# Two routings and a tail on one core: earlier and half strided gate matmuls, fewer warming transposes, and a bank of its own for the last logits group

## The reference

```python
# 1: linear attention, batch 4, 8 heads, 768 steps, head size 48
for t in range(S):
    cur = einsum('bhd,bhe->bhde', u * k[t], v[t])
    y[t] = einsum('bhd,bhde->bhe', r[t], state + cur)
    state = w * state + einsum('bhd,bhe->bhde', k[t], v[t])
# x: 3072 rows of 384
# 2: mixture of experts, E = 8, hidden 1024, for rows with x @ w_skip > 0 only
e = argmax(x @ w_gate); gate = softmax(x @ w_gate)[e]
x = x + gate * (relu(x @ w1[e]) @ w2[e])
# 3: a second such layer for every row, without the addition of x
out = gate * (relu(x @ w1b[e]) @ w2b[e])
```

## Time and profile before

| | us |
|---|---|
| median of 3 runs | 567.01 (564.94 to 568.14) |
| the profiled execution | 566.76 |
| its span, first to last instruction | 564.9 |
| TensorE busy | 535.0 |
| VectorE busy | 377.9 |
| ScalarE busy | 267.1 |
| GpSimd busy | 257.0 |

### The profile page before, as it was taken

The page is one execution under the profiler, slowest core; times in us unless marked ns, Lnnn a source line. Parts: engine busy times, 40 slices in busy tenths (PEclk is TensorE's granted clock), DMA queues, the critical chain, the costliest instruction groups (busy, mean ns, idle before and its releaser), DMA issues. The chain is left out here.

```text
span 564.9 us, 15988 instructions
## 1 busy us (share of the span) xinstructions
PE 535.0 (95%) x5511; PEld 506.8 (90%) x5512; DVE 377.9 (67%) x825; ACT 267.1 (47%) x718; POOL 257.0 (45%) x374
## 2 busy tenths in 40 slices
PE   4899999996899999999998899999999999999994
PEld 4789988994899999999986899999999999999993
DVE  4788888885698878888855646564756464647331
ACT  0333333333667656778743546362635452626230
POOL 5887787765145554444412342423332413324241
PEclk9999999996799999999998899999999999999998
DMA  9788889857278876784478524544454544111101
GB/s 154 130 179 161 162 161 173 164 192 275 84 247 266 259 231 188 240 263 131 117 233 297 189 71 149 167 149 143 164 173 150 166 142 159 38 48 42 41 2 41
DMA packets 114129, 89.59 MB, mean 159 GB/s; under 512 B 80672, under 2 KB 104931, under 8 KB 114080
## 3 DMA queue, kind: packets, MB, share of 16 engines
q1 hardware_dynamic: 105744, 73.96, 46.5%
q0 software_dynamic: 7776, 14.82, 9.5%
q10 hardware_dynamic: 560, 0.20, 0.2%
HBM read 80.44 MB, written 13.27 MB: 166 GB/s over the span
## 5 line engine op out<-in xcount | busy, mean ns | idle before, releaser
L777 DVE TENSOR_TENSOR w_lo<-w_raw,w_hi 128x384 fp32r<-128x384 f32 (+1 forms) x224 | 130.1, 608 | 4.8 <-ACT w_hi L772 3.6
L772 ACT CAST w_hi<-w_raw 128x384 fp32r<-128x384 f32 (+1 forms) x224 | 120.2, 566 | 4.2 <-issue 4.2
L1134 PE MATMUL e_ps_h<-e_x_hi,w_hi 128*128 128x192 f32 (+3 forms) x384 | 119.3, 311 | 1.0 <-DVE e_x_lo L1342 0.5
L1136 PE MATMUL e_ps_h<-e_x_hi,w_lo 128*128 128x192 f32 (+3 forms) x384 | 119.3, 311 | 0.0
L1135 PE MATMUL e_ps_h<-e_x_lo,w_hi 128*128 128x192 f32 (+3 forms) x384 | 119.3, 311 | 0.0
L1384 DVE SCALAR_TENSOR_TENSOR e_h_lo<-e_ps_h,e_h_hi 128x128 fp32r<-128x128 f32 (+1 forms) x192 | 70.4, 397 | 42.6 <-ACT e_h_hi L1290 36.0
L1134 PE MATMUL e_ps_y<-w_hi,e_h_hi 128*128 128x384 f32 x272 | 95.6, 352 | 0.0
L1136 PE MATMUL e_ps_y<-w_hi,e_h_lo 128*128 128x384 f32 x272 | 91.4, 336 | 0.0
L1135 PE MATMUL e_ps_y<-w_lo,e_h_hi 128*128 128x384 f32 x272 | 91.4, 336 | 0.0
L1134 PEld LDWEIGHTS e_ps_h<-e_x_hi,w_hi 128*128 128x128 f32 x384 | 72.7, 189 | 2.7 <-DVE e_x_lo L1342 1.4
L1135 PEld LDWEIGHTS e_ps_h<-e_x_lo,w_hi 128*128 128x128 f32 x384 | 72.7, 189 | 1.0
(11 more groups left out here) (208 smaller groups left out, 936.2 us busy)
## 6 DMA issues: line engine op xcount, KB each, us to landing
w_raw<-in_moe_w_dram SPq DMA_DIRECT2D x32, 1536.0 KB, 6.4
r_in<-in_r_dram SPq DMA_DIRECT2D x24, 192.0 KB, 3.2
k_in<-in_k_dram SPq DMA_DIRECT2D x24, 192.0 KB, 3.9
v_in<-in_v_dram SPq DMA_DIRECT2D x24, 192.0 KB, 3.9
x_rows<-rows SPq DMA_DIRECT2D x24, 192.0 KB, 3.4
w_raw<-x_rows SPq DMA_DIRECT2D x4, 768.0 KB, 8.7
e_late_x<-x_rows SPq DMA_DIRECT2D x2, 768.0 KB, 6.7
x_in<-x_rows,e_ent_in POOLq DMA_INDIRECT x33, 3.0
```

Source lines behind the costliest of these rows:

```text
L772: act.copy(self._of(self.hi1[par], self.hi2[par], n), self._of(self.raw1[par], self.raw2[par], n)).then_inc(self.hi_done[par], 1)
L777: eng.tensor_tensor(self._of(self.lo1[par], self.lo2[par], n), self._of(self.raw1[par], self.raw2[par], n), self._of(self.hi1[par], self.h ...
L1134: pe.matmul(o, s_hi, m_hi, start=(k == 0), stop=False)
L1136: return pe.matmul(o, s_lo, m_hi, start=False, stop=(k == last))
```

## The change

GpSimd's four fills move ahead of the constants. `stay_warm` has 2 turns in layer one and 3 in layer two in place of 6. VectorE makes the first half of `words_by_column` ahead of `starts`. ScalarE copies only this half into `gate_words`, which is half as large. TensorE's gate matmuls move ahead of its wait for `routed`; they begin with the second half of the tiles, read from `words_by_column` at a stride of 24 elements, and go on with the first half from `gate_words`. `start_spans` moves behind the turn of the second tile. In the tail the last group has halves of the bank `ps_y[1]` and a second `lT` tile; its `logitsT` stands directly behind that of the group before.

```diff
-        gate_words = sb("gate_words", [P, TILES, 3, NCOL], BF16)
+        gate_words = sb("gate_words", [P, TILES // 2, 3, NCOL], BF16)
...
+            if m == 0:
+                for row in fresh_rows:
+                    pool.memset(row[:], 0.0).then_inc(made, 1)
             exact = dict(allow_small_or_imprecise_dtypes=True)
...
             if m == 0:
-                for row in fresh_rows:
-                    pool.memset(row[:], 0.0).then_inc(made, 1)
...
-            stay_warm(pe, ident, ps_spare[:], 6)
+            stay_warm(pe, ident, ps_spare[:], 3 if m else 2)
...
-            for n, half in enumerate(HALVES):
-                act.wait_ge(gates_spread, n + 1)
-                act.copy(gate_words[:, half, :, :].rearrange("p i w c -> p i (w c)"), words_by_column[:, :, :, half].rearrange("p w c i -> p i (w c)")).then_inc(gates_aside, 1)
+            act.wait_ge(gates_spread, 1)
+            act.copy(gate_words[:].rearrange("p i w c -> p i (w c)"), words_by_column[:, :, :, HALVES[0]].rearrange("p w c i -> p i (w c)")).then_inc(gates_aside, 1)
...
+            def spread_gates(half):
+
+                wide = [P, 3, NCOL, half.stop - half.start]
+                dve.tensor_tensor(words_by_column[:, :, :, half], col_is[:, :, half].unsqueeze(1).to_broadcast(wide), pieces[:, :, half].unsqueeze(2).to_broadcast(wide), ALU.mult).then_inc(gates_spread, 1)
...
+            dve.wait_ge(gates_split, 5)
+            spread_gates(HALVES[0])
             if m == 0:
                 link(dve.tensor_tensor(over_short[:], seen[:, :, TILES - 1:TILES].to_broadcast([P, E, MOST]), short_limit[:].unsqueeze(1).to_broadcast([P, E, MOST]), ALU.is_gt))
...
-            dve.wait_ge(gates_split, 5)
-            for half in HALVES:
-                wide = [P, 3, NCOL, half.stop - half.start]
-                dve.tensor_tensor(words_by_column[:, :, :, half], col_is[:, :, half].unsqueeze(1).to_broadcast(wide), pieces[:, :, half].unsqueeze(2).to_broadcast(wide), ALU.mult).then_inc(gates_spread, 1)
+            spread_gates(HALVES[1])
             dve.wait_ge(starts_made, 5 if m == 0 else 4)
...
-            lT = sb("lT", [P, P])
+            lT = [sb(f"lT{n}", [P, P]) for n in range(2)]
...
+            ps_lT = lambda g: ps_y[1][:, 0:P] if g == XG else ps_x[0][:, 0:P]
+            ps_l = lambda g: ps_y[1][:, P:2 * P] if g == XG else ps_x[1][:, 0:P]
...
+            pe.wait_ge(gates_spread, 2)
+            for i in range(TILES // 2, TILES):
+                pe.matmul(ps_gates, row_hot[:, :, i], words_by_column[:, :, :, i], start=(i == TILES // 2), stop=False)
+            pe.wait_ge(gates_aside, 1)
+            for i in range(TILES // 2):
+                ins = pe.matmul(ps_gates, row_hot[:, :, i], gate_words[:, i, :, :], start=False, stop=(i == TILES // 2 - 1))
+            ins.then_inc(gates_placed, 1)
             pe.wait_ge(routed, 1)
-            start_spans(pe)
 
             for n in range(4):
                 pe.transpose(ps_h[n][:, P * WHOLE:P * WHOLE + P], ident[:], ident[:])
-            for n, some in enumerate(HALVES):
-                pe.wait_ge(gates_aside, n + 1)
-                for i in range(some.start, some.stop):
-                    ins = pe.matmul(ps_gates, row_hot[:, :, i], gate_words[:, i, :, :], start=(i == 0), stop=(i == TILES - 1))
-            ins.then_inc(gates_placed, 1)
             turn_x(0, 0)
...
                 turn_x(0, n)
+                if n == 1:
+                    start_spans(pe)
...
-                    if g:
+                    if 0 < g < XG:
                         pe.wait_ge(lT_out, g)
-                    else:
+                    elif g == 0:
                         pe.wait_ge(x_lo_done, X * units_run + X)
...
                 for g in range(XG + 1):
-                    logitsT(g)
+                    if g < XG:
+                        logitsT(g)
                     if g + 2 < XG + 1:
                         turn(g + 2)
+                    if g == XG - 1:
+                        logitsT(XG)
                     logits_of(g)
...
                 for g in range(XG + 1):
-                    logitsT_out(g)
+                    if g < XG:
+                        logitsT_out(g)
                     if g + 2 < XG + 1:
                         turned_copy(act, g + 2, 0)
+                    if g == XG - 1:
+                        logitsT_out(XG)
                     logits_out(g)
```

More of the change, by code:

```diff
@@ L717, in _ @@
             dve.tensor_copy(table[:, 0:NCOL, 0], ids[:]).then_inc(routed, 1)
-        return row_hot, gate_words, gates_aside, routed
+        return row_hot, words_by_column, gates_spread, gate_words, gates_aside, routed
 class Weights:
@@ L783, in wait_split, with moe @@
         eng.wait_ge(self.lo_done[k][par], (self.N1, self.N - self.N1)[k] * (pair + 1))
-def moe(nc, both, block, m, W, rows, out_rows, ident, USED, table, starts, x_in, y_rows, w_g, lg, ent_last, row_hot, gate_words, gates_aside, routed):
+def moe(nc, both, block, m, W, rows, out_rows, ident, USED, table, starts, x_in, y_rows, w_g, lg, ent_last, row_hot, words_by_column, gates_spread, gate_words, gates_aside, routed):
     tag = f"e{m}"
@@ L865, in moe @@
         pairs = E // 2
-        TILES, NCOL = gate_words.shape[1], gate_words.shape[3]
-        HALVES = [slice(0, TILES // 2), slice(TILES // 2, TILES)]
+        NCOL, TILES = words_by_column.shape[2:]
         gates_placed = sem("gates_placed")
@@ L1226, in logitsT @@
                         for b in range(SIZES[g]):
-                            ins = pe.matmul(ps_x[0][GW * b:GW * b + GW, 0:P], w_g[:, c, :], xT[g % 2][b][:, P * c:P * c + P], start=(c == 0), stop=(c == DC - 1), skip_group_check=True)
+                            ins = pe.matmul(ps_lT(g)[GW * b:GW * b + GW, :], w_g[:, c, :], xT[g % 2][b][:, P * c:P * c + P], start=(c == 0), stop=(c == DC - 1), skip_group_check=True)
                     ins.then_inc(lT_ready, 1)
@@ L1232, in logits_of @@
                     pe.wait_ge(lT_out, g + 1)
-                    if g:
+                    if 0 < g < XG:
                         pe.wait_ge(l_out, g)
-                    pe.transpose(ps_x[1][:, 0:P], lT[:], ident[:]).then_inc(l_ready, 1)
+                    pe.transpose(ps_l(g), lT[g == XG][:], ident[:]).then_inc(l_ready, 1)
                 turn(0)
@@ L1315, in logitsT_out @@
                     act.wait_ge(lT_ready, g + 1)
-                    act.copy(lT[:], ps_x[0][:, 0:P]).then_inc(lT_out, 1)
+                    act.copy(lT[g == XG][:], ps_lT(g)).then_inc(lT_out, 1)
                 def logits_out(g):
@@ L1322, in logits_out @@
                     dst = y_logits[:] if i is None else lg[:, BY * i:BY * i + BY, COL:COL + E]
-                    act.copy(dst, ps_x[1][:, 0:P].rearrange("p (b w) -> p b w", w=w_g.shape[2])[:, 0:SIZES[g], COL:COL + E]).then_inc(l_out, 1)
+                    act.copy(dst, ps_l(g).rearrange("p (b w) -> p b w", w=w_g.shape[2])[:, 0:SIZES[g], COL:COL + E]).then_inc(l_out, 1)
                 turned_copy(act, 0, 0)
```

## The result

The changed kernel takes 563.86 us (median of 5 runs, 562.42 to 564.08) against 567.01 of the kernel before, run beside it: a ratio (of the runs as a whole, not of the two medians) of 0.9947 with an interval of 0.9922 to 0.9972. Two later sets of runs of the same kernel gave 0.9914 [0.9874, 0.9955] and 0.9932 [0.9912, 0.9952]. So it is faster, by 3.2 us between the medians, about half of the 6.1 us that the sum promised. Its profiled execution took 563.98 us, 0.1 above its median, with a span of 562.3 where the kernel before has 564.9.

A forecast was written before the change was run, and what follows sets the result against it. TensorE, busy 95% of the span, bounds the kernel; gains lie in both routings and the tail. Terms -3.2 - 2.4 + 0.3 + 0.1 - 0.2 - 0.9 = -6.3, less 0.2 given back: -6.1, median 560.9 us; range 559.4 to 564.3.

The forecast's parts named there:

- the clock rival: The clock falls early or rises late in one layer, slowing routing and expert start: 562.5 to 564.3 us; chance 0.20.
- Part 1, layer one: Routing of layer one: fewer warming transposes bring the reduce from 149.75 to 146.5, bound by VectorE's list; -3.2 us.
- Part 1, layer two: Routing of layer two: fewer warming transposes bring the reduce from 321.81 to 319.4; -2.4 us.
- 11 at the lower and 13 at the higher clock: Layer two's 24 warming transposes: the clock rises among them, so they take 3.9 us and end at 315.05.
- the case that the text priced at 1.1: Layer two: the clock does not rise in the 24 transposes, L626 ends at 320.6, and the gain is 1.1 us.
- Part 2: Gate words half copied, half read strided at 0.21 and 0.245 us a matmul: hidden in layer one, +0.3 us in two.
- The slower rival: TensorE at 1.2 GHz reads strided tiles at half the rate: 575 us at most; chance 0.04.
- Part 3: Register loads behind the second turn, before layer one's first expert: between -0.1 and 0.8 us, taken as +0.1.
- I take the two to run side by side: Layer one: the register loads run beside the turn's 0.9 us; if not, it is 0.8 us more.
- Part 4: GpSimd's four fills ahead of the constants, for VectorE's L672 in layer one: between 0 and -0.5, taken as -0.2 us.
- Part 5: The tail: the last group's 24 matmuls no longer wait for the group before; last sum at 305.4 against 306.30, -0.9 us.
- the signs that the prediction named for being wrong: VectorE idle over 1 us before L716, a last turn awaiting no DMA, or clock 0.5 past an expert stage's first 2 us.

The follow-up runs named there:

- after: The profiled execution of the changed kernel, all parts of the change against the kernel before: 563.98 us, with a median of 563.86 us over its 5 runs.
- e12: The change itself again, unchanged, against the kernel before: median 562.92 us.
- e11: The change with the register loads ahead of TensorE's gate matmuls, a second look, against the kernel before: median 560.21 us.
- e1: The change as it is, measured once more against the kernel before: median 562.87 us.
- e3: The change with the register loads moved ahead of TensorE's gate matmuls, against the kernel before: median 559.84 us.
- e10: The kernel before with only the register loads moved behind the second turn of x: median 569.94 us, ratio 1.0058 to the kernel before.
- e2: The change with the register loads put back behind the wait for `routed`, against the kernel before: median 561.51 us.
- e8: The change with early register loads, but GpSimd's fills behind the constants as before: reduce of layer one at 12.50 us; no total time given.
- e7: The change with early register loads, but the tail as before: tail's end back at 4.60 us; no total time given.
- e4: The change with all 6 turns of warming transposes in both layers, against the kernel before: median 568.58 us.
- e15: Second look at the change with late loads and 16 instead of 8 transposes before the first expert: 10.16 us from reduce to expert; no separate total given.
- e5: The change with early register loads and 2 turns of warming transposes in layer two as well: 560.26 us, ratio 0.9897 to the kernel before.

## Why the prediction was half right

The forecast was 560.9 us, with 0.70 on 559.6 to 562.4; the 563.86 lies above that, in the stretch of the clock rival. By part:

- **Part 1, layer one: right.** -3.2 predicted, -3.68 measured, and -3.55 to -3.68 in every profile with the edit (12.4 to 12.5 against 16.1), VectorE's list being what ends last, as said. 16 transposes took 3.62 (3.5). The surplus is VectorE's operation over `den`, 0.20 instead of 0.66: it counts now that VectorE's list ends last.
- **Part 1, layer two: the low end.** -2.4 predicted, -1.26 in the first profile; -1.2 to -2.5 in the others with this edit. The step "11 at the lower and 13 at the higher clock" took the instant at which the clock rose from one profile. In after it did not rise in the 24, the case that the text priced at 1.1. It is a draw between profiles, 0 to 1.3 us, and I gave it too small a place.
- **Part 2: right.** 0.21 and 0.245 us a strided matmul predicted, 0.208 and 0.240 measured, and the cost in layer two is 0.1 to 0.2 of the 0.3 in the four profiles of the change. The slower rival (double price at the lower clock) is excluded: the twelve of layer two ran at 0.50 of the clock. The weighing of the Trainium skill, "TensorE: Matmul & The Clock Gate", section "Back-to-back issue gap", against L626 went the way of L626.
- **Part 3: wrong, and this is the step that failed.** "I take the two to run side by side" gave +0.1, with 0.8 as the bound if they did not. It is +1.0 (9.15 against 8.11 to 8.19), outside the bound. The loads did run beside the turn; the path was the wrong one. I took the 2.4 us from the last turn to the first product for the split of x, under which the loads would hide. They were the expert's own prologue on TensorE's queue (branches, moves and two more register loads, L915 and L916), which takes 2.3 us before and after alike, and the two loads now stand ahead of it. Their price was too low as well: 0.8 is the distance between the starts of two engines, on the queue it is 1.1. And the terms gave more than the bound: 2.7 less 2.4, and 0.8, are 1.1. The larger half is a consequence that had no term: TensorE stands still meanwhile, and the first expert runs at 1.2 GHz, 1.6 to 3.1 us in the four profiles of the change. Together it is 2.7 us between the medians of e12 and e11, 3.0 between e1 and e3, 3.3 by the ratio of e10, and only 1.4 between e1 and e2: about the missing half of the gain.
- **Part 4: too high.** At most 0.1 us by e8, whose reduce is at 12.50 with the old order and 12.39 to 12.51 with the new; 0.2 had been taken, from a single profile's 0.66.
- **Part 5: right.** -0.9 predicted, -0.86 in every profile with the edit, gone in e7.
- **The rivals.** The clock rival (0.20, 562.5 to 564.3) has the measured time in its range, and two of its terms came: 1.1 of its 1.3 us in L626 of layer two, and an expert stage that begins slow. The second had another mechanism: the rival blamed the fewer transposes, and e4 (all of them kept, clock low) and e2 (fewer, clock high) exclude that. I set "Against: the turns and transposes that raised it at 156.58, just before the experts, all stay". They stay, but the late loads put a gap between them and the expert. Of the signs that the prediction named for being wrong, two came: VectorE's 1.21 us before the reduce of layer two, and a granted clock of 0.50 up to 4 us into the first expert.
- **The sum without the failed step.** All of the change with the loads early came to 0.9885 and 0.9881, that is 6.5 and 6.7 us by the ratio and 7.6 and 6.3 between the medians, where the sum said 6.1.

The Trainium skill, "TensorE: Matmul & The Clock Gate", section "PE-mode transpose", has it that transposes do not count as busy for the clock. The kernel before speaks against it (the rise at 142.92 and 313.58 amid transposes alone), and so does e15: behind 3.65 us of sixteen transposes and nothing else the clock was high 0.4 us into the expert, where the change has it 4.0 to 6.6 us in.

Two kernels beat both the one before and the change: e3 at 559.84 and 560.21 us, and e5 at 560.26.

## What to carry to other kernels

An instruction that is moved off a busy path has to be costed against the queue that it lands in: name what comes behind it there, up to the first instruction that matters, the prologue of the next loop included. Where TensorE comes to a stage with a gap just ahead of it, add to the gap the price of the stage's first microseconds at the lower clock, here 1.6 to 3.1 us for idle times of 0.8 to 2.4 us in all, though one profile with 0.9 paid nothing. Where the profile says "issue", or names an engine that had long been done, read the register loads and branches of the engine's own queue by source line. Two shortenings can need each other: fewer transposes alone gave 0.9938, and the kernel with early loads 0.9885 with the strided gates and 0.9916 with copies, so test the parts together and apart.

## What the runs showed of the hardware

- Two register loads on TensorE's queue took 0.48 and 0.31 us, with their moves 1.1 us; the prologue of the first expert behind them 2.3 us, and the first product came 0.10 us after its last instruction. From the last turn's start to the product that is 3.4 us, and the profile marks the idle time (1.27 us in after) "issue".
- A strided bf16 moving tile (48 bytes apart) costs 0.208 us for 114 columns and 0.240 for 135 while the granted clock is 0.50, the same as the line through the earlier trace rows gave; L626 itself took 0.147 us for 76 columns at a clock of 1.0 and 0.149 in e11 at 0.50. The stride sets this price, not the clock.
- Stand-stills of 1.3 to 1.7 us marked "issue" inside straight runs of matmuls, in 5 of 19 profiles at one place, each with a late packet of the instruction queue q8.
- The clock rose or stayed low among the same 24 transposes from one execution to the next, worth up to 1.3 us before the reduce of layer two.
